# Dealing a group's four indirect scatter transfers over one turn of the loop

## What is computed

```python
for t in range(S):                       # attention, 4 x 8 heads, state 48 x 48
    y[:, :, t] = einsum('bhd,bhde->bhe', q[:, :, t], state)
    v_old = einsum('bhde,bhd->bhe', state, kt)
    state += bt * einsum('bhd,bhe->bhde', kt, vt - v_old)
x = ((x @ w1) * (x @ w2)) @ w3 @ w_out   # 3072 tokens, 384 -> 1024 -> 384
logits = x @ w_gate + modality_bias[modality_id]
e_idx = argmax(logits, axis=1)           # one expert a token
out[e_idx == e] = gate_w * (relu(x[e_idx == e] @ w1_e[e]) @ w2_e[e])
```

## Time and profile before

| what | value |
|---|---|
| median of 3 runs | 974.9 us (974.3 to 976.1) |
| the profiled execution's own time | 973.8 us |
| its span, first to last instruction | 971.9 us |
| TensorE matmul busy | 888.7 us (91%) |
| VectorE, ScalarE, GpSimd busy | 490.3, 343.2, 274.4 us |
| granted TensorE clock, mean | 0.965 of full speed |
| indirect scatters to the sorted rows | 24, 23.4 us of GpSimd |

### The profile page before, as it was taken

The page is one execution under the profiler, slowest core; times in us unless marked ns, Lnnn a source line. Parts: engine busy times, 40 slices in busy tenths (PEclk is TensorE's granted clock), DMA queues, the critical chain, the costliest instruction groups (busy, mean ns, idle before and its releaser), DMA issues.

```text
span 971.9 us, 29550 instructions
## 1 busy us (share of the span) xinstructions
PE 888.7 (91%) x11972; PEld 741.6 (76%) x11973; DVE 490.3 (50%) x891; ACT 343.2 (35%) x628; POOL 274.4 (28%) x296
## 2 busy tenths in 40 slices
PE   5999989999999999899989999996379999999996
PEld 4766657788778877787778778785269899999985
DVE  2567666665755576557654752233265333333332
ACT  1344444444544453345424532220243222222221
POOL 5345544443454344434434210011000111101010
PEclk9999989999999999999989999998679999999998
DMA  7424311111121111111111010101931111111110
GB/s 247 129 84 140 84 38 37 38 38 38 37 72 38 38 38 54 54 38 38 44 52 33 17 45 10 33 33 56 326 143 43 42 42 41 39 46 44 41 41 21
DMA packets 46570, 60.13 MB, mean 62 GB/s; under 512 B 9192, under 2 KB 39160, under 8 KB 45552
## 3 DMA queue, kind: packets, MB, share of 16 engines
q1 hardware_dynamic: 38640, 42.35, 14.5%
q0 software_dynamic: 3200, 9.56, 2.6%
q10 hardware_dynamic: 4608, 6.46, 2.3%
HBM read 42.26 MB, written 11.77 MB: 56 GB/s over the span
## 4 chain that ended last, share of the span: by engine, by line
PE 80%; DVE 5%; POOL 5%; issue 3%; ACT 3%; another core or an unknown queue 1%; DMA 1%; SPq 1%; ACTq 0%; DVEq 0%; POOLq 0%
PE banks L1427 19%; PE banks L1552 12%; PE banks L1445 11%; PE banks L1566 11%; PE banks L1288 4%; PE banks L1397 3%; PE banks L1355 3%; PE banks L1583 2%; PE banks L1365 2%; PE banks L1248 2%; PE banks L1377 2%; POOL nm L543 1%; PE banks L1344 1%; POOL inv L547 1%
## 5 line engine op out<-in xcount | busy, mean ns | idle before, releaser
L1427 PE MATMUL banks<-xr,w12r 128*128 128x512 f32 x864 | 227.9, 412 | 7.6 <-DVE xr L941 7.5
L1427 PEld LDWEIGHTS banks<-xr,w12r 128*128 128x128 f32 x864 | 161.0, 194 | 45.5 <-issue 9.5
L1552 PE MATMUL banks<-experts,kept 128*128 x486 | 124.5, 411 | 11.0 <-DVE experts L1180 8.5
L1552 PEld LDWEIGHTS banks<-experts,kept 128*128 128x128 f32 x486 | 92.6, 195 | 32.4 <-issue 11.7
L1566 PE MATMUL banks<-experts,kept 128*128 x624 | 114.8, 340 | 0.0
L1445 PE MATMUL banks<-kept,hr 128*128 128x392 f32 x576 | 112.2, 347 | 0.0
L1566 PEld LDWEIGHTS banks<-experts,kept 128*128 128x128 f32 x624 | 107.1, 188 | 0.0
L1445 PEld LDWEIGHTS banks<-kept,hr 128*128 128x128 f32 x576 | 100.9, 188 | 2.0
L594 POOL DMA_INDIRECT out<-ys,xs x26 | 25.6, 984 | 259.7 <-DVE ys L1215 259.7
L531 POOL TENSOR_TENSOR kb<-keys,beta_sb 128x384 f32<-128x384 f32 x24 | 29.1, 1213 | 244.4 <-PE banks L1387 244.4
L874 DVE TENSOR_TENSOR picked<-inv,masks_sb 128x512 f16<-128x512 f16 x96 | 47.0, 489 | 77.0 <-ACT inv L630 76.0
(11 more groups left out here) (144 smaller groups left out, 1318.7 us busy)
## 6 DMA issues: line engine op xcount, KB each, us to landing
raw<-in_moe_w SPq DMA_DIRECT2D x6, 1536.0 KB, 7.3
kq<-in_qT SPq DMA_DIRECT2D x24, 256.0 KB, 2.7
xs<-sorted_rows ACTq DMA_DIRECT2D x28, 197.0 KB, 2.4
kraw<-in_k SPq DMA_DIRECT2D x24, 192.0 KB, 2.4
vals<-in_v SPq DMA_DIRECT2D x48, 96.0 KB, 2.5
w3T<-in_w3T SPq DMA_DIRECT2D x8, 512.0 KB, 4.3
w<-in_w SPq DMA_DIRECT2D x8, 384.0 KB, 4.2
xT<-yT SPq DMA_DIRECT2D x48, 64.0 KB, 2.1
```

The source lines that it names most:

```text
L1427: last = mm(psum[:, UP + w, :], w12r[:, p, w, k, j * P:(j + 1) * P], xr[:, r, k, :], start=(k == 0 and p == r), stop=(k == KT - 1 and p == 1))
L1552: last = mm(psum[:, f, :], xsr[:, w, p, k, :], experts[:, bass.ds(slot * (2 * WE) + at, FF // 2)], start=(k == 0 and p == r), stop=(k == K ...
```

## The change

`scatter` gets a list of tiles. In its turn the transfers of tiles 0, 1 and 2 each wait for one more semaphore, `x_taken[2]`, `x_taken[3]` and `x_taken[4]`, which ScalarE increments as it has evicted the pair products of that level. The transfer of tile 3 is moved behind `beta_keys`. Where no unit is live (turns 24 and 28), the waits on `x_taken` are left out.

```diff
-            def scatter(c):
+            def scatter(c, tiles=range(B)):
                 pool.wait_ge(q["place_ready"], c + 1)
                 pool.wait_ge(q["row_ready"], c + 1)
                 alone(pool)
-                for t in range(B):
+                for t in tiles:
                     nc.gpsimd.indirect_dma_start(
...
                     if piece and piece[0] and piece[1] == RANK:
-                        scatter(piece[0] - 1)
+                        for level in range(2, LV):
+                            if live(u):
+                                pool.wait_ge(x_taken[level], u + 1)
+                            scatter(piece[0] - 1, [level - 2])
                 if live(u + 1):
                     beta_keys(u + 1)
+                for at in range(SPLITS):
+                    piece = piece_of(u - 1, at)
+                    if piece and piece[0] and piece[1] == RANK:
+                        scatter(piece[0] - 1, [LV - 2])
                 if live(u + 2):
                     normalise(u + 2)
```

## The result

| | before | after |
|---|---|---|
| median, lowest to highest | 975.4 us (974.3 to 976.1, 4 runs) | 961.9 us (960.1 to 963.6, 4 runs) |
| the profiled execution, its span | 973.8, 971.9 us | 961.1, 959.3 us |
| granted TensorE clock, mean | 0.965 | 0.972 |
| turns 12, 16, 20 | 27.62, 27.53, 28.90 us | 22.90, 22.74, 22.71 us |
| the turns behind them (13, 17, 21) | 23.13, 23.11, 23.11 us | 23.95, 23.80, 23.71 us |

The ratio is 0.9862, with 0.984 to 0.9884 as its 95% interval. The lines behind 590 have moved by eight: L630 is L638 now, L893 is L901, L1288 is L1296, and so on.

What follows compares the result with a forecast made beforehand. TensorE bounds quiet turns; in turns 12, 16 and 20 its messages arrive late beside scatter bursts. 973.8 less 15.95, plus 1.65 and 0.3, is 959.8 us; with 1.1 for the median, 960.9 us, range 957.5 to 970.

Steps and rivals of the forecast that it cites:

- The first step: Turns 12, 16, 20: scatter bursts make TensorE's messages late; dealing them removes the whole 15.95 us excess, clock included.
- What a lone scatter costs: Beside chain steps in turns 12, 16, 20: one scatter delays a TensorE message 1.28 us, bounds 0 and 3.94.
- Tiles 0 and 1: Beside level 3 and level 4: covers of 1.32 and 0.87 us leave costs of 0 and 0.41 us a turn.
- Tile 3: Beside `scores`, L1273 and L1291: delay reaches TensorE through VectorE's L865, cover 1.14 us, cost 0.14 us a turn.
- GpSimd's queue: Around L531 and L513: L531 0.3 us late, tile 3 fits 1.90 us idle, cost 0; without room or cover 1.6 a turn.
- Turn 24: Burst stays there; added waits on three transfers, all already met, may lose 0.3 us.
- Rival 1: Three covered places, turns 12, 16, 20: a lone scatter costs 2.15 us, 9.4 us in all, 968.4 us; chance 0.15.
- Rival 3: Same turns: each lone scatter delays messages 3.94 us, so slower, 984.4 us; decides from 2.88 us on; chance 0.07.
- Rival 4: Tiles 2 and 3, 2.7 us apart: two scatters still meet, 8 us of gain lost, 967 us; chance 0.03.
- Rival 2: Turns 12, 16, 20: scatter cost is only moved, or the excess has another cause; no change, 974.9 us; chance 0.10.

Runs made afterwards that it cites:

- `dense_slots`: Kernel before, with turns 12, 16 and 20's scatters each at a long dense piece's start (tile 0 behind `square`, tile 3 ahead of `beta_keys`): 962.4 us, ratio 0.9878, chip 9.
- `dose`: Kernel before, with one, two and three scatters left at the old place in turns 12, 16 and 20, the rest behind `final_done` and `y_done`: 957.9 us, chip 0.
- `after_again`: The changed kernel as it stands, run again on chip 9 beside the kernel before (974.6 us): 961.9 us, ratio 0.9861.
- `pair_at_final`: Kernel before, with tile 0 behind `error_done`, 1 and 2 behind `final_done`, 3 behind `y_done`, turn 24 dealt too: 956.0 us, ratio 1.0, chip 11.
- `extra_direct`: Kernel before, with four additional plain whole-row transfers from GpSimd's queue at the old place, real scatters later: 957.5 us against 955.4, chip 0.

## Why the prediction was right

**What is late.** The first step holds: with the burst dealt, the three turns read 22.9, 22.7 and 22.7 us at a clock of 1.00, and 15.70 of the 15.95 us of the earlier trace rows are gone, the part that I had charged to the clock included. That GpSimd's transfers cause it is shown on chip 1 within one kernel: two at the old place cost 0.55 us, four (of 8 floats a row) 4.9. What stays open is the path on the chip. The rows show late semaphore events and a TensorE that halts at "issue" beside scatters; they don't show what holds them. The sentence of the Trainium skill that I had put against the change ("SBUF — State Buffer", section "Who interferes with whom": "PE and ACT never wait on anyone.") would, as I read it, have left the time at 974.9 us, and it did not stay there. The trace has TensorE halting beside scatters, 0.51 us inside L1299; whether that goes against a section on ports, no run here shows.

**What a lone scatter costs.** I took 1.28 us and had 0 to 3.94 as bounds. The answers were 0.34 to 0.56 us late beside tiles 0 and 1, and 1.14, 0.42 and 0.43 us beside tile 3, so 1.28 us was above all of them. Tiles 0 and 1 were to cost 0.41 us a turn; turns 12, 16 and 20 lie 0.20, 0.04 and 0.01 above the quiet 22.70, so 0.25 us for 1.23. They are also about 1 us later than I had placed them: `x_taken[2]` comes at 288.46 + 0.59 = 289.05 and the scatter starts at 290.04.

**Tile 3, the step that was mis-sized.** I had 0.14 us a turn, through VectorE's L865 with 1.14 us of cover. It costs 0.82, 0.69 and 0.60 us, 2.1 us in all for 0.4. The path that I had was the wrong one: L873 is late by 1.14 us in turn 13 and by 0.42 and 0.43 in turns 17 and 21, less than the cover, and these turns are long as well. TensorE halts by itself, 0.51, 0.51 and 0.49 us, with 60 short matmuls in 1.7 us ahead of it in turn 13, and cover on VectorE is no protection against that. The whole loss of turn 13 stands there: counted from `scores`, the dense piece behind L1299 starts at 2.38 us and at 1.52 in the kernel before, and from it to the turn's end the changed kernel loses nothing more. In `dense_slots`, with the fourth scatter 2 us earlier, beside a dense piece, turns 13, 17 and 21 are at 23.11. That run also takes the scatter from behind `beta_keys` and from tile 2's, so which of the two neighbours makes it costly is not separated.

**GpSimd's queue, a step that came right by luck.** "L513 still ended by L857" was wrong: L513 follows the scatter without idle time. I had L531 late by 0.3 us; it ends 23.61 us into turn 12 and 22.42 into turn 8, so it is 1.2 us late (0.2 of it TensorE's own): the third transfer starts 0.84 us behind its increment, which I had at nothing, and then takes 1.79 us. The room that I counted, 1.90 us, was filled, and GpSimd's `square` of turn 13 is late by 1.05 us (8.92 us into the turn against 7.87), that of turn 17 by 0.67. I had looked for the cover at L906 (1.85 us). The reader that counts is VectorE's L855, as `dose` shows, and there the cover is 0.53 us. That this cost nothing is because TensorE was 0.84 us late already at L1299.

**Turn 24.** I gave the waits that are already met 0.3 us. The stretch from L1281 to L1309 is 6.27 us against 5.53 before, but it is 6.24 against 6.22 on chip 9, so the waits cost nothing and the difference is between executions. Another such difference is the clock behind the halt: the nine matmuls there take 2.34 us in the changed kernel and 3.91 in `after_again`, most of the 2.0 us between their last columns. What I missed is that this turn still held 3 to 4 us.

**The sum.** -15.70, +2.1 in turns 13, 17 and 21, +0.5 behind the last `scores` (415.7 against 415.2) and +0.7 ahead of turn 12 (it starts at 276.26, and 275.57 before) make -12.4 us; the span went from 971.9 to 959.3, by 12.6. The last two terms are differences between executions as far as chip 9 tells them apart from the change. The forecast for the profiled execution was 959.8 us and it took 961.1. That it was so near is in part luck: tile 3 cost 1.7 us more than I had, the other two terms 0.9 more, and tiles 0 and 1 cost 1.0 less. The larger luck is the chip, since on three of the five known here there was no excess to take away.

**The rivals.** Rival 1 needed 2.15 us for a lone scatter; none above 1.14 was seen. Rival 3 needed 2.88. Rival 4 had scatters 2.7 us apart as too close; tiles 2 and 3 start 2.8 us apart, and 2.1 us in all are lost there, not 8; in part it may be right, as said of tile 3. Rival 2, no change, failed on chip 9 and in the first comparison. On chips 0, 11 and 14 the kernel before has no excess to take away, so no gain is to be had there. The changed kernel was not run on them. An estimate for them: at least the 0.67 us by which `square` is late in turn 17, less the cover of 0.53, and at most the 0.63 us of `dose`, in each of three turns, so 0.4 to 2 us slower.

## What to carry to other kernels

Where GpSimd makes indirect transfers beside a chain of many short matmuls, deal them out singly and put each at the start of a long dense piece, away from VectorE instructions that get longer beside GpSimd's. (All of this together, as in `pair_at_final`, was not run where messages come late.) The number in a row and the place count, their size doesn't, and a halt of TensorE at "issue" is not covered by slack on the engine that reads its result. Compare such variants on one chip only, and look first whether the effect occurs on it: seven of the twelve runs here fell on chips that didn't have it, and could answer nothing about it.

## What the runs showed that I had not expected

- Chips differ by 2%, all or nothing: 955.4 to 955.9 us on three, 974.6 to 975.4 us on two and in the first comparison. Why is open; by the length of their turns, the four with a burst are all that tells them apart.
- Four transfers of 8 floats a row delay TensorE's messages as much as four of 394 (27.62 and 27.6 us for the turn).
- The delay grows faster than the burst: 0 to 1.1 us for one, 0.8 and 1.4 for two, 2.8 and 3.6 for four. The cost grows faster still, since only with four at the old place the clock falls too.
- A wait of VectorE for GpSimd (L855 for `square`) lets GpSimd's lateness through to TensorE with 0.53 us of cover, where I had counted 1.85 at another reader.
- A VectorE instruction of 0.17 us takes 1.25 us beside a scatter and L531, one of 0.43 us takes 0.77 beside L522 and 2.02 beside a scatter and L522.
- Whether plain transfers from GpSimd's queue have the effect is not known: `extra_direct` ran on chip 0 alone. `pair_at_final` on a chip with late messages wasn't run.
